# Attention in pairs of heads: the next pair's first and left-over scores ahead of the last pair's transposes

## The chip, the cores and the metric

One core of one Trainium2 chip runs the whole program. The metric is the device time of one execution in microseconds (us). Before the change it was 721.33 us, the median of three runs (720.55 to 721.36). For this kernel a difference of about 0.2%, 1.44 us, is what a measurement can tell from no change.

## What is computed

```python
def reference(q, k, v, U, V, w1, w2, w_in, w_sp, b_sp, w_out):     # B=4, H=8, S=576, D=64
    s = (q @ k.T) / sqrt(D) - slope[h] * abs(i - j)                # kept for 0 <= i - j < 128, else -1e9
    x = softmax(s) @ v                                             # heads side by side: (B, S, 512)
    u = x + (x.T @ U @ V).T                                        # mixing over the sequence, rank 32
    y = u + relu(u @ w1) @ w2                                      # 512 -> 2048 -> 512
    a, g = split(relu(y @ w_in))                                   # 512 -> 2 x 512
    return (a * (w_sp @ norm(g) + b_sp)) @ w_out
```

The change concerns the first line of it and the work woven into it: the attention with its window of 128 keys.

## The kernel before

The program is written engine by engine: five instruction streams, each in a fixed order of its own, with semaphores between them. Nothing reorders them. PE is the tensor engine, DVE the vector engine, ACT the scalar engine, POOL the gpsimd engine, SP the queue that issues the DMAs.

The attention goes in 16 steps, one for each pair of heads of each of the four batches, numbered p = 0 to 15 here (`step(b, i)` with p = 4b + i, from L1833 on PE and from L1312 on DVE; batches 2 and 3 are a hardware loop). A pair's 576 queries are cut into nine score tiles, `TILE_ORDER`: tiles 0 to 3 (blocks 0 and 1 of both heads) come from `scores_x`, tile 4 (the left-over 64 queries of both heads in one tile) from `scores_z`, tiles 5 to 8 from `scores_y`, which writes into the same two PSUM banks as `scores_x`. `scores_x` and `scores_y` use two halves of 64 rows of the PE array side by side; `scores_z`, the transposes and the mixing use all of its rows and columns; `values` uses two halves of 64 columns.

For each tile DVE adds the bias, takes the row's minimum of the negated scores and writes the tile to `sc` (`score`, L1258), and ACT takes the exponential (L927). PE then transposes the tiles in four groups of four (`turn` with f = 0 to 3, L1757). The groups use two PSUM banks in turn: f = 0 and 2 use bank 3, f = 1 and 3 use bank 4. DVE copies groups 0, 1 and 3 out (`keep_pt`, L1267), ACT copies group 2 (L936), and `turn` 2 and 3 wait for the copies of 0 and 1. `values` (L1774, L1781) multiplies the copies by v, `turn_back` (L1792) and `turn_x` (L1804) turn the result twice, with DVE dividing by the sums in between (`normalise`, L1288 and L1291). `mix_up` (L1827, L1828) and, once a batch, `mix_down` (L1813, L1814) do the low-rank mixing; `mix_up` uses the banks of the transposes and so waits for their copies. In the step after a `mix_down`, DVE has one more instruction, `lo_t` (L1298), ahead of `normalise`.

The work is staggered: a step p holds the scores of pair p, the transposes and `values` of pair p-1, and `turn_back`, `normalise` and `turn_x` of pair p-2. In the order of the code a step on PE before is: `turn` 0, `turn` 1 (p-1), `scores_x`, `scores_z` (p), `turn` 2 (p-1), `turn_back` (p-2), `turn` 3 (p-1), `scores_y` (p), `turn_x` (p-2), `mix_up`, `values` (p-1). On DVE it is: copies 0 and 1 (p-1), `score` tiles 0 to 3 (p), `lo_t` where there is one, `normalise` (p-2), copy 3 (p-1), `score` tiles 4 to 8 (p), the additions of the mixing, the sums.

The waits that matter are: `scores_x` waits until DVE has read all nine tiles of the pair before, since it writes over them; `scores_y` waits until DVE has read tiles 0 to 3 of its own pair, for the same reason; DVE's tile 0 waits for `scores_x`.

After the attention come the two large products (L1916 to L1918 and L1958 to L1960) and the second block (from L2027), in which PE is never without work for long.

Of the kernel before, what the change touches and what calls it, by code (L numbers as in the profile page):

```python
# [54 lines left out]
AFTER_X, AFTER_Z = 4, 5  # L55
# [70 lines left out]
def program(nc, qk, v_n, mu, mv, w1, w2, w_in, w_sp, b_sp, w_out, out_t, u_scr, r_scr, w2_scr, x2_scr, wc_scr):  # L126
    ctx = ExitStack()
    with ctx:
# [1110 lines left out]
        def _(dve):  # L1239
            def score(b, i, ns):  # L1240

                p, s = b * PAIRS + i, i % 2
                for n in ns:
                    t, e = TILE_ORDER[n]
                    if n in (0, AFTER_X, AFTER_Z):
                        dve.wait_ge(qk_done, 3 * p + (0, AFTER_X, AFTER_Z).index(n) + 1)
                    if n == 0 and not (isinstance(b, int) and p < 2):
                        dve.wait_ge(tr_done, 4 * (p - 1))
                    if n in (0, AFTER_X, AFTER_Z):
                        dve.sem_inc(dve_passed, 1)  # L1250
                    if e is None:
                        src, add, out = z_ps[:, 0:TAILKEYS], tbias[:, i, :], sc[:, s, n, 0:TAILKEYS]
                    elif t == 0:
                        src, add, out = s_ps[e][:, 0:P], bias[:, 2 * i + e, P:KEYS], sc[:, s, n, P:KEYS]
                    else:
                        c = {1: P, 2: 0, 3: KEYS}[t]
                        src, add, out = s_ps[e][:, c:c + KEYS], bias[:, 2 * i + e, :], sc[:, s, n, :]
                    dve.tensor_tensor_reduce(out=out, in0=src, in1=add, scale=-SCALE, scalar=3e38, op0=ALU.add,  # L1258
                                             op1=ALU.min, accum_out=mn[:, s, n:n + 1]).then_inc(scored, 1)

            def keep_pt(b, i, f):

                p = b * PAIRS + i
                dve.wait_ge(tr_done, 4 * p + f + 1)
                if f == 0 and not (isinstance(b, int) and p == 0):
                    dve.wait_ge(pv_done, p)
                dve.tensor_copy(pt[:, f % 2, f // 2 * BANK:(f // 2 + 1) * BANK],  # L1267
                                pt_ps[f % 2][:, :]).then_inc(pt_kept, 1)
# [43 lines left out]
            def step(b, i):  # L1312
                whole = not isinstance(b, int)
                one, two = whole or b * PAIRS + i >= 1, whole or b * PAIRS + i >= 2
                ago, k = MIX_STEP[i]
                if one:
                    keep_pt(*back(b, i, 1), 0)
                    keep_pt(*back(b, i, 1), 1)
                score(b, i, range(0, AFTER_X))
                if i == 2 and (whole or b >= 1):  # L1320
                    lo_t(b - 1)
                if two:
                    normalise(*back(b, i, 2))
                if one:
                    keep_pt(*back(b, i, 1), 3)
                score(b, i, range(AFTER_X, NT))
                if whole or b >= ago:
                    add_u(b - ago, k, pt_ps)
                if one:
                    sums(*back(b, i, 1))  # L1330
# [380 lines left out]
        def _(pe):  # L1711
            def scores_x(b, i):

                p, s = b * PAIRS + i, i % 2
                pe.wait_ge(qk_in[s], 32 * (b * 2 + i // 2 + 1))
                if not (isinstance(b, int) and p == 0):
                    pe.wait_ge(scored, p * NT)
                for t in (0, 1):
                    for e in range(2):
                        half = slice(e * D, (e + 1) * D)  # L1720
                        o = s_ps[e][:, 0:P] if t == 0 else s_ps[e][:, P:P + KEYS]
                        last = pe.matmul(o, qkraw[half, s, S + t * P:S + (t + 1) * P],  # L1722
                                         qkraw[half, s, 0:P if t == 0 else KEYS], start=True, stop=True)
                last.then_inc(qk_done, 1)

            def scores_z(b, i):

                s = i % 2
                pe.matmul(z_ps[:, 0:TAILKEYS], qkraw[:, s, S + (TILES - 1) * P:2 * S + TAIL],
                          qkraw[:, s, S - TAILKEYS:S], start=True, stop=True).then_inc(qk_done, 1)  # L1730
# [13 lines left out]
            def turn(b, i, f, mixed=None):  # L1744

                p = b * PAIRS + i
                pe.wait_ge(exp_done, p * NT + FILL_TILES[f])
                if f == 0 and not (isinstance(b, int) and p == 0):
                    pe.wait_ge(pt_third, p)
                elif f == 1 and not (isinstance(b, int) and p == 0):  # L1750
                    pe.wait_ge(pt_kept, 3 * p)
                elif f >= 2:
                    pe.wait_ge(pt_kept, 3 * p + f - 1)
                if f < 2 and mixed is not None:
                    pe.wait_ge(u_kept, mixed)
                for j, (n, w) in enumerate(FILLS[f]):
                    last = pe.transpose(pt_ps[f % 2][:, j * P:(j + 1) * P], sc[:, i % 2, n, w * P:(w + 1) * P],  # L1757
                                        ident[:, :])
                last.then_inc(tr_done, 1)
# [70 lines left out]
            def back(b, i, n):  # L1830
                return (b, i - n) if i >= n else (b - 1, i - n + PAIRS)

            def step(b, i):  # L1833
                whole = not isinstance(b, int)
                p = b * PAIRS + i
                one, two = whole or p >= 1, whole or p >= 2
                ago, k = MIX_STEP[i]
                last_ago, last_k = MIX_STEP[(i - 1) % PAIRS]
                last_ago += i == 0
                mixed = HEADROOM + (b - last_ago) * 2 * KD + 2 * last_k + 2 if whole or b >= last_ago else None  # L1840
                if one:
                    turn(*back(b, i, 1), 0, mixed)
                    turn(*back(b, i, 1), 1, mixed)
                scores_x(b, i)
                scores_z(b, i)
                if one:
                    turn(*back(b, i, 1), 2)
                if two:
                    turn_back(*back(b, i, 2))
                if one:  # L1850
                    turn(*back(b, i, 1), 3)
                scores_y(b, i)
                if two:
                    turn_x(*back(b, i, 2))
                if whole or b >= ago:
                    pe.wait_ge(pt_third, p)
                    pe.wait_ge(pt_kept, 3 * p)
                    mix_up(b - ago, k, pt_ps)
                if one:
                    values(*back(b, i, 1))  # L1860
                if i == 1 and (whole or b >= 1):
                    mix_down(b - 1)
# [280 lines left out]
```

## Time and profile before

| | us |
|---|---|
| median of three runs | 721.33 |
| the profiled execution, its time | 721.14 |
| its span, first to last instruction | 719.4 |
| PE busy | 708.4 |
| DVE busy | 452.4 |
| ACT busy | 339.0 |
| POOL busy | 179.6 |

The attention takes the first 137 us or so of the span. The timelines merge neighbouring instructions of one line into one row; the first number is the start, the second the time from the first one's start to the last one's end, and the ends of matmuls are modelled, so that the next row often starts before the last has ended. An fp32 matmul of the code stands as two in the trace. The distance between two starts is what a piece of work costs PE.

### The profile page before, as it was taken

To read this page: it belongs to the slowest core of one execution; us is meant where nothing else is said; L and a number is where in the kernel's file an instruction comes from. 1 tells how busy PE (TensorE), PEld (TensorE's weight loads), DVE (VectorE), ACT (ScalarE), POOL (GpSimd) and SP (SyncE) were. 2 spreads that over 40 slices of the span, in tenths; PEclk is the share of its full clock that TensorE was granted. 3 is DMA by queue.
4 is the path that set the end of the run, shared out by engine and by line. 5 is a ranking of instruction groups with operands and counts; after the bars stand their busy time and mean duration, and the time that the engine had idled before them with its cause. 6 is when DMAs were issued, how large, how long until landed. Compare 5 with 4: busy or idle time off the path is not lost.

```text
span 719.4 us, 13038 instructions
## 1 busy us (share of the span) xinstructions
PE 708.4 (98%) x4656; PEld 663.3 (92%) x4656; DVE 452.4 (63%) x1032; ACT 339.0 (47%) x764; POOL 179.6 (25%) x184
## 2 busy tenths in 40 slices
PE   8999999999999999999999999999999999999998
PEld 5677777799999999999999999999898998998997
DVE  6978787788673265248878976976384454354341
ACT  6878788865352243334444444444352432432422
POOL 2598646510009806660050000000010100100100
PEclk9999999999999999999999999999999999999999
DMA  7669974055457855899286175468900100100101
GB/s 224 192 212 389 355 262 144 16 177 189 176 171 260 300 205 181 285 370 374 87 277 220 44 264 176 149 208 301 335 1 1 67 0 0 66 0 0 66 1 67
DMA packets 72145, 122.46 MB, mean 170 GB/s; under 512 B 4896, under 2 KB 43808, under 8 KB 71584
## 3 DMA queue, kind: packets, MB, share of 16 engines
q1 hardware_dynamic: 72096, 121.82, 49.0%
q8 instruction: 29, 0.48, 0.3%
q14 instruction: 20, 0.16, 0.1%
HBM read 74.29 MB, written 47.51 MB: 169 GB/s over the span
## 4 chain that ended last, share of the span: by engine, by line
PE 74%; DVE 4%; ACT 0%; issue 0%; DVEq 0%
PE bank L1916 8%; PE bank L1918 8%; PE bank L1917 8%; PE bank L1958 4%; PE bank L1960 4%; PE bank L1959 4%; PE wide L1958 3%; PE wide L1960 3%; PE wide L1959 3%; PE bank L2067 2%; PE bank L2069 2%; PE bank L2068 2%; PE bank L1883 2%; PE bank L1881 2%; PE bank L1882 2%; PE wide L1882 2%
## 5 line engine op out<-in xcount | busy, mean ns | idle before, releaser
L1916 PE MATMUL bank<-xs,w1s 128*128 128x384 f32 x336 | 113.0, 336 | 1.0 <-DVE tok L1440 0.8
L1918 PE MATMUL bank<-xs,w1s 128*128 128x384 f32 x336 | 112.3, 334 | 0.0
L1917 PE MATMUL bank<-xs,w1s 128*128 128x384 f32 x336 | 112.3, 334 | 0.0
L1073 ACT ACTIVATE rk<-tok 128x768 fp32r<-128x768 f32 x72 | 61.0, 849 | 71.1 <-PE bank L1960 32.4
L914 POOL TENSOR_TENSOR vl<-vr,vh 128x512 fp32r<-128x512 f32 x8 | 11.2, 1405 | 291.8 <-ACT vh L1198 291.8
L1051 ACT ACTIVATE sums_u<-bank 128x384 f32<-128x384 f32 x72 | 35.3, 491 | 89.8 <-PE bank L1918 89.5
L927 ACT ACTIVATE sc<-sc,mn 128x256 f32<-128x256 f32 (+1 forms) x144 | 67.0, 468 | 19.7 <-DVE mn L1258 19.7
L1958 PE MATMUL bank<-rk,w2q 128*128 128x384 f32 x208 | 69.9, 336 | 0.2 <-DVE rk L1462 0.2
L1959 PE MATMUL bank<-rk,w2q 128*128 128x384 f32 x208 | 69.5, 334 | 0.0
L1960 PE MATMUL bank<-rk,w2q 128*128 128x384 f32 x208 | 69.5, 334 | 0.0
L1916 PEld LDWEIGHTS bank<-xs,w1s 128*128 128x128 f32 x336 | 63.1, 188 | 2.7 <-issue 1.3
L1917 PEld LDWEIGHTS bank<-xs,w1s 128*128 128x128 f32 x336 | 63.1, 188 | 0.0
L1918 PEld LDWEIGHTS bank<-xs,w1s 128*128 128x128 f32 x336 | 63.1, 188 | 0.0
L1462 DVE TENSOR_TENSOR rk<-tok,rk 128x768 fp32r<-128x768 f32 x48 | 46.8, 978 | 14.0 <-ACT rk L1073 13.6
L1258 DVE CUSTOM_DVE_ANT_0 sc<-bank,bias 128x256 f32<-128x256 f32 (+1 forms) x128 | 42.2, 384 | 5.8 <-PE bank L1722 4.9
L1958 PE MATMUL wide<-rk,w2q 128*128 128x384 f32 x128 | 42.9, 335 | 0.0
L1960 PE MATMUL wide<-rk,w2q 128*128 128x384 f32 x128 | 42.8, 334 | 0.0
L1959 PE MATMUL wide<-rk,w2q 128*128 128x384 f32 x128 | 42.8, 334 | 0.0
L1267 DVE COPY pt<-bank 128x512 f32<-128x512 f32 x48 | 31.4, 682 | 14.7 <-PE bank L1757 14.6
L1958 PEld LDWEIGHTS bank<-rk,w2q 128*128 128x128 f32 x208 | 39.0, 188 | 1.2 <-DVE rk L1462 1.1
L1959 PEld LDWEIGHTS bank<-rk,w2q 128*128 128x128 f32 x208 | 39.0, 188 | 0.0
L1960 PEld LDWEIGHTS bank<-rk,w2q 128*128 128x128 f32 x208 | 39.0, 188 | 0.0
(216 smaller groups left out, 1839.3 us busy)
## 6 DMA issues: line engine op xcount, KB each, us to landing
r_scr<-tok SPq DMA_DIRECT2D x20, 768.0 KB, 3.8
tok<-r_scr SPq DMA_DIRECT2D x15, 768.0 KB, 6.8
w1raw<-w SPq DMA_DIRECT2D x32, 256.0 KB, 4.1
w2q<-w_scr SPq DMA_DIRECT2D x4, 2048.0 KB, 10.3
wc_scr<-wprep SPq DMA_DIRECT2D x12, 512.0 KB, 6.5
w_scr<-tok SPq DMA_DIRECT2D x11, 512.0 KB, 3.1
qkraw<-qk SPq DMA_DIRECT2D x16, 320.0 KB, 4.9
qkraw<-qk SPq DMA_DIRECT2D x16, 288.0 KB, 3.5
```

The lines of the kernel that those rows point to most:

```text
L927: act.activation(w, w, ACT.Exp, bias=mn[:, s, n:n + 1], scale=-1.0, accum_out=sm[:, i, c:c + 1]).then_inc(exp_done, 1)
L1051: act.activation(sums_u[:, i, :], a_ps[s % 2][:, 0:HT], ACT.Copy).then_inc(kept, 1)
L1073: act.activation(rk[:, n % RING, 0], raw(g, RAW_OF[m])[:, 2 * j:2 * j + 2, :], ACT.Relu if m <= 3 else ACT.Copy).then_inc(rk_hi, 1)
L1258: dve.tensor_tensor_reduce(out=out, in0=src, in1=add, scale=-SCALE, scalar=3e38, op0=ALU.add, op1=ALU.min, accum_out=mn[:, s, n:n + 1]).th ...
L1267: dve.tensor_copy(pt[:, f % 2, f // 2 * BANK:(f // 2 + 1) * BANK], pt_ps[f % 2][:, :]).then_inc(pt_kept, 1)
L1462: dve.tensor_tensor(lo, x, hi, ALU.subtract).then_inc(rk_lo, 1)
L1916: pe.matmul(o, wh, ah, start=(k == 0 and m in FRESH), stop=False, skip_group_check=True)
L1917: pe.matmul(o, wl, ah, start=False, stop=False, skip_group_check=True)
L1918: last = pe.matmul(o, wh, al, start=False, stop=(k == 1), skip_group_check=True)
L1958: pe.matmul(o, wh, rh, start=(kk == 0 and m in FRESH), stop=False, skip_group_check=True)
L1959: pe.matmul(o, wl, rh, start=False, stop=False, skip_group_check=True)
L1960: last = pe.matmul(o, wh, rl, start=False, stop=(kk == UNITS - 1), skip_group_check=True)
```

## The change

On PE, `scores_x` and `scores_z` of the step now stand ahead of the transposes of the pair before, and `turn` 2 stands behind `turn_back`. On DVE, `score` of tiles 0 and 1 stands ahead of the first two copies, and tiles 2 and 3 stay behind them. ACT, POOL and SP have the same instructions in the same order, and none is added or removed but a few register instructions of the loop.

```diff
@@ DVE, step
                 ago, k = MIX_STEP[i]
+                score(b, i, range(0, 2))
                 if one:
                     keep_pt(*back(b, i, 1), 0)
                     keep_pt(*back(b, i, 1), 1)
-                score(b, i, range(0, AFTER_X))
+                score(b, i, range(2, AFTER_X))
@@ PE, step
+                scores_x(b, i)
+                scores_z(b, i)
                 if one:
                     turn(*back(b, i, 1), 0, mixed)
                     turn(*back(b, i, 1), 1, mixed)
-                scores_x(b, i)
-                scores_z(b, i)
-                if one:
-                    turn(*back(b, i, 1), 2)
                 if two:
                     turn_back(*back(b, i, 2))
                 if one:
+                    turn(*back(b, i, 1), 2)
                     turn(*back(b, i, 1), 3)
                 scores_y(b, i)
```

PE in step 7, from `values` of one step to `turn_x` of the next, before (L1757 are the transposes of the scores, L1722 is `scores_x`, L1729 `scores_z`, L1739 `scores_y`):

```order
L1757 MATMUL bank<-ident,sc 128x128 x8
L1722 MATMUL bank<-qkraw 128x128 x2
L1722 MATMUL bank<-qkraw 128x256 x2
L1729 MATMUL bank<-qkraw 128x192
L1757 MATMUL bank<-ident,sc 128x128 x4
L1792 MATMUL wide<-ident,xt 128x128 x4
L1792 MATMUL wide<-ident,xt 64x128
L1757 MATMUL bank<-ident,sc 128x128 x4
L1739 MATMUL bank<-qkraw 128x256 x4
L1804 MATMUL wide<-ident,xn 128x128 x5
```

The same in the changed kernel, where each of these lines has a number one higher:

```order
L1723 MATMUL bank<-qkraw 128x128 x2
L1723 MATMUL bank<-qkraw 128x256 x2
L1730 MATMUL bank<-qkraw 128x192
L1758 MATMUL bank<-ident,sc 128x128 x8
L1793 MATMUL wide<-ident,xt 128x128 x4
L1793 MATMUL wide<-ident,xt 64x128
L1758 MATMUL bank<-ident,sc 128x128 x8
L1740 MATMUL bank<-qkraw 128x256 x4
L1805 MATMUL wide<-ident,xn 128x128 x5
```

The three rows of scores moved to the front, and the second and third group of transposes now stand together behind `turn_back`.

DVE in step 6, the one after the first `mix_down`, before (COPY is `keep_pt`, L1258 with a bank is `score`, L1298 `lo_t`, L1288 the start of `normalise`):

```order
L1267 COPY pt<-bank 128x512 x2
L1258 ISA sc,mn<-bank,bias 128x128
L1258 ISA mn 128x1
L1258 ISA sc,mn<-bank,bias 128x128
L1258 ISA mn 128x1
L1258 ISA sc,mn<-bank,bias 128x256
L1258 ISA mn 128x1
L1258 ISA sc,mn<-bank,bias 128x256
L1258 ISA mn 128x1
L1298 TENSOR_TENSOR tst<-wide,tst 64x512
L1288 TENSOR_TENSOR xn<-wide,rinv 128x512
```

The same in the changed kernel:

```order
L1258 ISA sc,mn<-bank,bias 128x128
L1258 ISA mn 128x1
L1258 ISA sc,mn<-bank,bias 128x128
L1258 ISA mn 128x1
L1267 COPY pt<-bank 128x512 x2
L1258 ISA sc,mn<-bank,bias 128x256
L1258 ISA mn 128x1
L1258 ISA sc,mn<-bank,bias 128x256
L1258 ISA mn 128x1
L1298 TENSOR_TENSOR tst<-wide,tst 64x512
L1288 TENSOR_TENSOR xn<-wide,rinv 128x512
```

The first two scores stand ahead of the two copies; the other two stay directly ahead of `lo_t` and `normalise`.

PE in step 1, the second pair, where there is no pair p-2 yet; first before, from `scores_y` of step 0 on:

```order
L1739 MATMUL bank<-qkraw 128x256 x4
L1757 MATMUL bank<-ident,sc 128x128 x8
L1722 MATMUL bank<-qkraw 128x128 x2
L1722 MATMUL bank<-qkraw 128x256 x2
L1729 MATMUL bank<-qkraw 128x192
L1757 MATMUL bank<-ident,sc 128x128 x8
L1739 MATMUL bank<-qkraw 128x256 x4
```

And in the changed kernel:

```order
L1740 MATMUL bank<-qkraw 128x256 x4
L1723 MATMUL bank<-qkraw 128x128 x2
L1723 MATMUL bank<-qkraw 128x256 x2
L1730 MATMUL bank<-qkraw 128x192
L1758 MATMUL bank<-ident,sc 128x128 x16
L1740 MATMUL bank<-qkraw 128x256 x4
```

The first eight transposes, which stood ahead of the second pair's scores, now stand behind them, and all sixteen follow each other.

## Rows read from the trace of the kernel before

**Rows 1.** The page, its head: span and instructions.

```profile
span 719.4 us, 13038 instructions
```

**Rows 2.** Busy time by stretch: us, PE, PEld, DVE, ACT, POOL, clock, DMA share, GB/s.

```profile
9.00:33.00 24.00, 21.63 (x196) 16.02 (x194) 22.87 (x93) 20.60 (x74) 8.75 (x10) 1.00 0.66 203
33.00:137.00 104.00, 103.60 (x902) 80.65 (x897) 83.38 (x336) 85.29 (x278) 68.86 (x59) 1.00 0.71 244
...
144.00:719.00 575.00, 570.32 (x3493) 557.33 (x3492) 338.35 (x574) 224.55 (x399) 93.21 (x97) 1.00 0.45 157
```

**Rows 3.** Timeline of PE, plain step: start us, us, engine, line, operation, operands.

```profile
101.71 1.09 PE L1757 MATMUL bank<-ident,sc 128*128 128x128 f32 x8
102.74 0.93 PE L1722 MATMUL bank<-qkraw 64*128 64x128 f32 x8
103.59 0.59 PE L1729 MATMUL bank<-qkraw 128*128 128x192 f32 x2
104.02 0.60 PE L1757 MATMUL bank<-ident,sc 128*128 128x128 f32 x4
104.46 0.71 PE L1792 MATMUL wide<-ident,xt 128*128 128x128 f32 x5
105.00 0.60 PE L1757 MATMUL bank<-ident,sc 128*128 128x128 f32 x4
105.53 1.14 PE L1739 MATMUL bank<-qkraw 64*128 64x256 f32 x8
...
107.12 0.38 PE L1827 MATMUL bank<-mvh,tst 128*128 128x288 f32 x1
...
109.71 0.55 PE L1757 MATMUL bank<-ident,sc 128*128 128x128 f32 x3
```

**Rows 4.** Timeline of DVE, same step; in brackets idle time and what ended it.

```profile
102.41 1.29 DVE L1267 COPY pt<-bank 128x512 f32<-128x512 f32 x2 [0.48 <-PE bank L1757]
103.97 0.29 DVE L1258 CUSTOM_DVE_ANT_0 sc<-bank,bias 128x128 f32<-128x128 f32 x1 [0.27 <-PE bank L1722]
...
104.74 0.42 DVE L1258 CUSTOM_DVE_ANT_0 sc<-bank,bias 128x256 f32<-128x256 f32 x1
105.09 0.08 DVE L1258 DVE_READ_ACCUMULATOR2_ANT mn<- 128x1 f32 x1
105.44 0.69 DVE L1288 TENSOR_TENSOR xn<-wide,rinv 128x512 f32<-128x512 f32 x1 [0.27 <-PE wide L1792]
...
106.24 0.67 DVE L1267 COPY pt<-bank 128x512 f32<-128x512 f32 x1
```

**Rows 5.** Timeline of DVE in the step after `mix_down`.

```profile
88.84 0.69 DVE L1298 TENSOR_TENSOR tst<-wide,tst 64x512 fp32r<-64x512 f32 x1
89.57 0.69 DVE L1288 TENSOR_TENSOR xn<-wide,rinv 128x512 f32<-128x512 f32 x1
```

**Rows 6.** Timeline of PE in that step.

```profile
85.48 1.03 PE L1757 MATMUL bank<-ident,sc 128*128 128x128 f32 x8
...
90.50 0.76 PE L1804 MATMUL wide<-ident,xn 128*128 128x128 f32 x5
```

**Rows 7.** Timeline of PE, second pair's step.

```profile
11.06 0.93 PE L1722 MATMUL bank<-qkraw 64*128 64x128 f32 x8 [0.35 <-DVE mn L1258]
...
13.43 1.13 PE L1739 MATMUL bank<-qkraw 64*128 64x256 f32 x8
```

**Rows 8.** Timeline of DVE, second to fourth step.

```profile
14.77 0.42 DVE L1258 CUSTOM_DVE_ANT_0 sc<-bank,bias 128x256 f32<-128x256 f32 x1 [0.38 <-PE bank L1739]
...
17.58 1.29 DVE L1267 COPY pt<-bank 128x512 f32<-128x512 f32 x2
...
26.95 1.29 DVE L1267 COPY pt<-bank 128x512 f32<-128x512 f32 x2
...
29.39 0.08 DVE L1258 DVE_READ_ACCUMULATOR2_ANT mn<- 128x1 f32 x1
```

**Rows 9.** Timeline of PE, fourth step: scores that had waited for DVE.

```profile
29.52 1.13 PE L1739 MATMUL bank<-qkraw 64*128 64x256 f32 x8
```

## The prediction

> **What bounds the kernel now.** I read the span [rows 1], then the busy time by stretch [rows 2]. From 33 to 137 us PE is busy 103.60 of 104 us and DVE 83.38: the attention's steady part is bound by PE. From 9 to 33 us DVE is busy 22.87 of 24 us and PE 21.63: there DVE sets the pace. Behind 144 us PE is busy 570.32 of 575 us with work that the change doesn't touch. So the attention's length goes into the total nearly one for one, and the question is what a step costs after the change.
>
> Next the timelines of one plain step. A step before takes 109.71 - 101.71 = 8.00 us, and no PE row of it names a wait [rows 3]. DVE in the same step has two holes, 0.48 us ahead of the first copies and 0.27 us ahead of the first score [rows 4]. DVE's last score of tiles 0 to 3 ends at 105.09 + 0.08 = 105.17, and PE needs it for `scores_y`, which starts at 105.53: a cover of only 0.36 us. That cover is where the change bites.
>
> **The change part by part, plain step.** I count from U, the start of `scores_x`, which now opens the step.
>
> PE's own time up to `scores_y`, by distances between starts [rows 3]: `scores_x` 0.85, `scores_z` 0.43, four transposes 0.44, four more 0.44, `turn_back` 0.54, four transposes 0.44, and the last four with the passage to the half-array scores 0.53. Sum 3.67. Before, `scores_y` stood 105.53 - 101.71 = 3.82 behind the step's start. The 0.15 saved is one passage between forms of matmul: `values` (64 columns), transposes (whole array), `scores_x` (64 rows) were two passages; `values` to `scores_x` is one. The trace has no passage from 64 columns to 64 rows. From below its cost beyond normal spacing is zero, from above the two that it replaces, about 0.25 (a passage costs about 0.1 where I can read it: 0.53 for the last four transposes against 0.44). I take the same 0.1, because both known kinds cost that.
>
> Row and rule: the rows show a later start at every passage between forms. The Trainium skill, "TensorEngine Tiling (Array Packing)", section Key Properties, says that changing the tiling mode drains the TensorE, whichever tile is used; by that rule alone, one passage fewer in a step, the change would be a gain, and the rows agree with the rule. What it leaves out is the wait that follows.
>
> DVE's chain in the same step. Tiles 0 and 1 can start when `scores_x` is through: U + 0.93, and DVE starts 0.30 later (102.74 + 0.93 = 103.67 against 103.97) [rows 3, 4], so U + 1.23. The two take 0.43 (104.74 less 103.97, less one of 0.35 for tile 2) and end at U + 1.66. The first copy needs transpose group 0: 0.85 + 0.43 + 0.60 = U + 1.88, plus 0.05 from transposes to copy (half of the eight of 101.71 ends at 102.36, the copy starts at 102.41), so U + 1.93. DVE idles 0.27 here. Two copies occupy 2 x 0.61 (the pair of 1.29 less one of 0.67 is the distance) [rows 4]: tile 2 starts at U + 3.14, tile 3 at 3.48, its end with the accumulator's read is at 3.83 + 0.08 = U + 3.91. PE answers DVE's end after 0.05 (29.39 + 0.08 against 29.52) [rows 8, 9]. So `scores_y` starts at **U + 3.96**: 0.29 later than PE could, and 0.14 later than before. The cover of 0.36 has become a wait, since copies 0 and 1, which ran while PE did `scores_x`, now stand between `scores_x` and tiles 2 and 3.
>
> Behind `scores_y` everything on PE keeps its distances, if nothing else is late. `mix_up` would start 107.12 - 105.53 = 1.59 later, at U + 5.55. It needs the third copy: `normalise` starts near U + 3.9, the copy 0.80 later, and it lasts 0.67 [rows 4], so U + 5.37: in time by 0.18. The earlier start of ACT's exponentials of tiles 0 and 1 buys nothing: ACT's copy of group 2 waits for transposes that come at U + 3.1, and tile 4's exponential stands behind work that waits for `turn_x`. A plain step costs **+0.14**. There are seven with `mix_up` (7 to 9, 11 to 13, 15): +0.98. Steps 4 and 5 without it have the same chain up to `scores_y`; one of them loses a small wait, so +0.23 for both.
>
> **The step after a `mix_down`** (6, 10 and 14). Before, it starts at 85.48, and `turn_x` at 90.50, 5.02 later, comes 0.93 after the start of `normalise` (89.57), which comes 0.73 after `lo_t` (88.84) [rows 5, 6]. It already hangs on DVE. No passage is saved here, because `mix_down` uses the whole array: `scores_x` starts 0.09 behind the point where the transposes stood. Then tile 3 ends as above at 3.83 (accumulator's start), `lo_t` 0.12 later, `normalise` + 0.73, `turn_x` + 0.93: 0.09 + 3.83 + 0.12 + 0.73 + 0.93 = 5.70, against 5.02: +0.68. The 0.12 may vanish or not (it stands between the read and `lo_t` and is idle), so 0.56 to 0.68. I take 0.65, three times: **+1.95**.
>
> **The start.** Step 1's `scores_x` waits for DVE's ninth score and starts at 11.06 either way [rows 7]. Before, the first eight transposes and DVE's copies of them were done beside that wait. After, transposes start at 11.06 + 1.28 = 12.34, the first copy at 12.34 + 0.65 = 12.99, tile 2 at 14.20, tile 3 ends at 14.97, `scores_y` starts at 15.02, against 13.43 [rows 7]: +1.59. DVE's next scores follow 1.34 behind `scores_y` (14.77 against 13.43) [rows 7, 8], so all of it passes on. In step 2, DVE is free at 17.58 + 1.59 = 19.17 [rows 8] and again waits 0.27 between its first scores and first copy, which costs some 0.2 more; in step 3 it is free long after PE (26.95, [rows 8]), the order of its work doesn't matter, and 0.1 comes back. Sum for steps 1 to 3: **+1.68**.
>
> Total: 1.68 + 0.23 + 1.95 + 0.98 = **+4.84 us**. Behind step 15 the tail has its old order, and the 575 us that follow are PE's. The profiled execution took 721.14 us for a span of 719.4, 0.19 below the median of 721.33. So 721.14 + 4.84 = 725.98; I give 726.0.
>
> **Rivals.**
>
> Not slower: the passage decides. If DVE's chain kept up, PE would gain 0.15 to 0.2 in the twelve steps whose predecessor ends with `values`, 1.8 to 2.4 us, against the start's 1.7: 721.14 - 0.7 to 721.14 - 0.1, about 720.7. For this, tile 3 must end at U + 3.62 and not at 3.91. Against it: the 1.88 to the end of group 0 and the 1.22 of the copies are plain rows. I give 0.09, a third of it faster by over 0.2%.
>
> Milder: the plain steps break even (the new passage costs nothing), and `lo_t` follows at once: 1.5 + 3 x 0.5 = 3.0, less what a step may gain; 722.8 to 724.2. Chance 0.10.
>
> Dearer: the register instructions that the loop puts between tile 1 and the first copy, or the third copy with its cover of 0.18, hold up every step by a further 0.3: twelve steps, +3.6, 729.6. Chance 0.06.
>
> The clock: a step would have 21 transposes in a row, 2.4 us; the granted clock is 1.00 in every stretch of the attention, 2.4 GHz, with eight in a row [rows 2]. If it fell to 1.2 GHz in each such run, a run would at most double: 15 x 2.4 = +36, 757. Nothing in the rows speaks for it, and PE does the same work in between; chance 0.01. The Trainium skill, "TensorE: Matmul & The Clock Gate", Part 4, says that matmuls in transpose mode don't count as a busy PE for the clock; no row here shows such a fall.
>
> That the change does something else than it says is out: the order of the instructions shows it.
>
> **How the numbers follow.** The forecast has 0.74, with its own range of 724.3 to 728.4: from below, +3.3 (a free passage at the nine plain steps and 0.2 less at the start and at `lo_t`); from above, +7.2 (a passage of 0.2, and 0.1 of register work, in twelve steps). The range that should hold the time 8 times in 10 takes part of the milder rival: 723.4 to 728.6. A measurement of this kernel tells 0.2%, 1.44 us, from no change. Slower by more: 0.91 (forecast, dearer, clock, milder). Within: 0.06. Faster by more: 0.03.
>
> **What the profile after would show.** In a plain step of 8.14 us, a wait of PE for DVE's `mn` ahead of `scores_y`, which starts 3.96 behind `scores_x`; DVE idle 0.3 us between tile 1 and the first copy, and about 1 us ahead of tile 0; `turn_x` in steps 6, 10 and 14 some 5.6 behind `scores_x`, with a wait for `xn`; `scores_y` of step 1 at 15.0. The attention's end, the first large product, some 4.8 us later than before, and the same distances from there on. I am wrong if `scores_y` stands at U + 3.7, if the start is made up in steps 2 and 3, or if PE's waits behind the attention shrink.

## The result, and the profile after

The changed kernel takes **728.07 us** (median of four runs, 726.98 to 729.25) against 721.35 (720.55 to 722.18) of the kernel before, measured beside it: a ratio of 1.0096, with a 95% interval of 1.0082 to 1.011. It is slower by 0.8 to 1.1%, and the forecast of 726.0 in 723.4 to 728.6 holds the time, near its upper end. The profiled execution took 726.98 us.

The page's head and the busy time by stretch, columns as in [rows 2]:

```profile
span 725.2 us, 13044 instructions
```

```profile
9.00:33.00 24.00, 21.10 (x168) 15.80 (x169) 20.47 (x80) 18.90 (x65) 8.77 (x10) 0.93 0.59 186
33.00:137.00 104.00, 101.83 (x871) 77.36 (x870) 80.11 (x327) 82.99 (x267) 67.35 (x58) 1.00 0.72 247
```

The span is 5.8 us longer than in [rows 1], and PE's instructions are the same but for their order. In the stretch from 33 to 137 us PE is busy 101.83 us where it was 103.60 [rows 2]: it now waits where it didn't. The first stretch has a clock of 0.93, where before it was 1.00.

The plain step of PE that answers to [rows 3]:

```profile
97.86 0.93 PE L1723 MATMUL bank<-qkraw 64*128 64x128 f32 x8
...
101.81 1.13 PE L1740 MATMUL bank<-qkraw 64*128 64x256 f32 x8
...
106.00 0.93 PE L1723 MATMUL bank<-qkraw 64*128 64x128 f32 x8
```

`scores_y` stands 101.81 - 97.86 = 3.95 behind `scores_x`, and the step takes 106.00 - 97.86 = 8.14 us, where it took 8.00. DVE in the same step, answering to [rows 4]:

```profile
99.09 0.29 DVE L1258 CUSTOM_DVE_ANT_0 sc<-bank,bias 128x128 f32<-128x128 f32 x1 [0.99 <-PE bank L1723]
...
99.78 1.29 DVE L1267 COPY pt<-bank 128x512 f32<-128x512 f32 x2 [0.19 <-PE bank L1758]
...
101.67 0.08 DVE L1258 DVE_READ_ACCUMULATOR2_ANT mn<- 128x1 f32 x1
```

DVE is idle 0.99 us ahead of tile 0 and 0.19 ahead of the copies; tile 3's read ends at 101.67 + 0.08 = 101.75, and `scores_y` starts 0.06 later. The idle time of PE ahead of the line of `scores_y`, over the whole attention: 5.5 us in 15 waits (from the view of that line):

```profile
  DVE mn L1258: 5.5, 15
```

That is 1.0 us in the first pair's step, which is in the kernel before too, and some 0.3 us in each of fourteen others.

The step after a `mix_down` (step 10), DVE and then PE, answering to [rows 5, 6]:

```profile
92.99 0.69 DVE L1298 TENSOR_TENSOR tst<-wide,tst 64x512 fp32r<-64x512 f32 x1
93.72 0.69 DVE L1288 TENSOR_TENSOR xn<-wide,rinv 128x512 f32<-128x512 f32 x1
```

```profile
89.06 0.93 PE L1723 MATMUL bank<-qkraw 64*128 64x128 f32 x8
...
94.65 0.77 PE L1805 MATMUL wide<-ident,xn 128*128 128x128 f32 x5 [0.50 <-DVE xn L1291]
```

`turn_x` starts 94.65 - 89.06 = 5.59 behind `scores_x`, 0.93 behind the start of `normalise` (93.72), which is 0.73 behind `lo_t`.

The start, PE in step 1, answering to [rows 7], and the busy time there in stretches of 2 us:

```profile
10.34 0.93 PE L1723 MATMUL bank<-qkraw 64*128 64x128 f32 x8 [1.81 <-DVE mn L1258]
...
11.62 3.71 PE L1758 MATMUL bank<-ident,sc 128*128 128x128 f32 x16
15.26 1.14 PE L1740 MATMUL bank<-qkraw 64*128 64x256 f32 x8
...
18.22 0.93 PE L1723 MATMUL bank<-qkraw 64*128 64x128 f32 x8
```

```profile
9.00:11.00 2.00, 0.66 (x8) 0.55 (x8) 1.19 (x8) 1.81 (x7) 0.00 (x0) 1.00 0.89 264
11.00:13.00 2.00, 2.00 (x13) 1.79 (x10) 0.83 (x5) 1.15 (x6) 0.00 (x0) 0.66 0.96 343
13.00:15.00 2.00, 1.98 (x10) 1.47 (x9) 1.74 (x6) 0.36 (x1) 0.00 (x0) 0.50 0.09 33
```

This isn't in the forecast. The granted clock falls to 0.50, the lower of the two levels, from 11.66 to 15.07 us in the record of the clock, and the sixteen transposes take 3.71 us. Before it, PE had been idle for 1.81 us, up to 10.34, in a stretch in which it had little work anyway.

The waits of PE, longest sums first (line waited at, what for, us in total, times, longest):

```profile
PE wide L1805 <- DVE xn L1291: 2.1, 4, 0.6
...
PE wide L1793 <- ACT xt L945: 1.0, 3, 0.5
```

The three waits for ACT's `xt` lie in steps 2, 3 and 4; that of step 4 is the longest, 0.47 us.

### The profile page after: what moved, and what is told of

Same layout as the page of the kernel before. It is cut to its first block, busy times and chain, and to the rows that moved or that the text cites. A ratio compares the mean times of both kernels' runs of the same rounds, so it can differ in the third digit from the quotient of the medians.

```text
span 725.2 us, 13044 instructions
## 1 busy us (share of the span) xinstructions
PE 711.0 (98%) x4656; PEld 663.5 (91%) x4656; DVE 450.7 (62%) x1032; ACT 340.6 (47%) x764; POOL 179.6 (25%) x184
## 4 chain that ended last, share of the span: by engine, by line
PE 73%; DVE 5%; ACT 0%; issue 0%; DVEq 0%; ACTq 0%
PE bank L1916 8%; PE bank L1918 7%; PE bank L1917 7%; PE bank L1958 4%; PE bank L1960 4%; PE bank L1959 4%; PE wide L1958 3%; PE wide L1960 3%; PE wide L1959 3%; PE bank L2067 2%; PE bank L2069 2%; PE bank L2068 2%; PE bank L1883 2%; PE bank L1881 2%; PE bank L1882 2%; PE wide L1882 2%
## 5 line engine op out<-in xcount | busy, mean ns | idle before, releaser
L1258 DVE CUSTOM_DVE_ANT_0 sc<-bank,bias 128x256 f32<-128x256 f32 (+1 forms) x128 | 43.3, 383 | 24.2 <-PE bank L1723 21.8
L1758 PE MATMUL bank<-ident,sc 128*128 128x128 f32 x256 | 37.2, 285 | 1.4 <-ACT sc L927 1.0
```

## Where the time went

A step's length is the distance between the starts of two steps: of `scores_x` after the change, and before it of `turn` 0 (in step 1 of `scores_x` there too). In the steps behind a `mix_down` the table counts, as the prediction did, the 0.09 us by which `scores_x` now starts later behind `mix_down`; "difference" is what all steps of a row lose together, in us:

| part | before | after | difference | forecast |
|---|---|---|---|---|
| up to `scores_x` of step 1 | 11.06 | 10.34 | -0.72 | 0 |
| step 1, `scores_x` to the next step | 5.33 | 7.88 | +2.55 | +1.59 |
| step 2 | 7.48 | 7.76 | +0.28 | +0.2 |
| step 3 | 9.31 | 9.26 | -0.05 | -0.1 |
| step 4 | 7.65 | 8.02 | +0.37 | } +0.23 |
| step 5 | | | +0.13 | } |
| steps 6, 10, 14 | | | +0.54, +0.65, +0.63 | 3 x 0.65 |
| steps 7 to 9, 11 to 13, 15 (a plain one takes) | 8.00 | 8.13 | +0.95 | +0.98 |
| up to the first large product | 143.96 | 149.31 | +5.35 | +4.84 |
| behind it | 575.44 | 575.89 | +0.45 | 0 |

The first row is no effect of the change. The first pair's `scores_x`, which has the same place in both kernels, took 1.65 us in the trace of before and 0.93 in that of after:

```profile
4.91 1.65 PE L1722 MATMUL bank<-qkraw 64*128 64x128 f32 x8
```

```profile
4.90 0.93 PE L1723 MATMUL bank<-qkraw 64*128 64x128 f32 x8
```

1.65 us is also what these matmuls take in a stretch with a clock of 0.50, and the record of the clock explains it. Its first entry, of 1.00, begins at 6.70 us in the trace of before and at 4.83 in that of after. Ahead of that entry nothing is recorded, and the views print 1.00 there all the same. In the fourteen traces of this case the entry begins between 4.74 and 7.32 us, and these matmuls take the longer the later it begins: 0.93 us up to 4.89, then 1.04 (5.18), 1.19 (5.50), 1.28 (5.69), 1.52 (6.16), and 1.65 from 6.47 on. So the row is the moment at which the full clock was granted, which differs from one execution to the next.

## The experiments

All kernels are the changed kernel with one or two edits, unless said otherwise; ratios are against the kernel before on the same chip.

**Step 1 in the old order.** Does the start cost what the sum says, and is the half clock part of it?

```diff
@@ PE, step
+                early = not whole and p == 1
+                if early:
+                    turn(*back(b, i, 1), 0, mixed)
+                    turn(*back(b, i, 1), 1, mixed)
                 scores_x(b, i)
                 scores_z(b, i)
-                if one:
+                if one and not early:
@@ DVE, step
-                score(b, i, range(0, 2))
+                early = not whole and b * PAIRS + i == 1
+                if not early:
+                    score(b, i, range(0, 2))
...
-                score(b, i, range(2, AFTER_X))
+                score(b, i, range(0 if early else 2, AFTER_X))
```

> The changed kernel with step 1 alone (the second pair) in the order of before, on PE and on DVE. Theory: the start costs 1.6 us by itself (scores and copies that no longer run beside the wait for DVE's ninth score) and some 1 us by a stretch of TensorE clock 0.50 that follows PE's idle time there. Both go: the clock is 1.00 throughout, the step's scores_y starts about 2.4 us behind its scores_x, and the time is before + 3.5 us (7 plain steps x 0.14, 3 steps after mix_down x 0.62, steps 4 and 5 together 0.5), about 724.9. Rival: the loss sits in the steady steps alone and the slow clock is chance: no better than before + 6.

Measured: 724.84 us (723.96 to 725.91, five runs), ratio 1.0055 (1.0041 to 1.0069). PE in step 1:

```profile
10.29 0.93 PE L1725 MATMUL bank<-qkraw 64*128 64x128 f32 x8 [0.36 <-DVE mn L1258]
...
12.66 1.13 PE L1742 MATMUL bank<-qkraw 64*128 64x256 f32 x8
...
15.62 0.93 PE L1725 MATMUL bank<-qkraw 64*128 64x128 f32 x8
```

`scores_y` is 2.37 behind `scores_x` and the next step begins 5.33 behind it, as before; the clock is 1.00 in all five runs. All later steps have the lengths of the changed kernel. Against the kernel before on its own chip this one loses 724.84 - 721.13 = 3.7 us, the changed kernel 6.7. So some 3.0 us of the loss lie in step 1 and 3.7 in the rest, where the forecast had 1.59 and 3.25.

**Only PE's order changed**, DVE's old one (both copies, then all four scores):

```diff
@@ DVE, step
-                score(b, i, range(0, 2))
                 if one:
                     keep_pt(*back(b, i, 1), 0)
                     keep_pt(*back(b, i, 1), 1)
-                score(b, i, range(2, AFTER_X))
+                score(b, i, range(0, AFTER_X))
```

> The new order on PE, the old order on DVE (two copies, then tiles 0 to 3). Theory: DVE's chain decides; tile 0 starts at U + 3.14 (U: start of scores_x), tile 3 ends at U + 4.34, scores_y starts at U + 4.39, a plain step takes 8.56 us, and the time is some 6 us above the changed kernel's, 733 to 735. Rival: what costs is PE's new order by itself (another passage between forms of matmul, more waits of turn_back): a plain step stays at 8.13 and the time at 728.

Measured: 733.97 us (a single run). A plain step of PE:

```profile
65.88 0.93 PE L1722 MATMUL bank<-qkraw 64*128 64x128 f32 x8
...
70.25 1.13 PE L1739 MATMUL bank<-qkraw 64*128 64x256 f32 x8 [0.39 <-DVE mn L1258]
...
74.43 0.93 PE L1722 MATMUL bank<-qkraw 64*128 64x128 f32 x8
```

`scores_y` stands at U + 4.37, the step takes 8.55, where adding the same rows in another order had given 4.39 and 8.56. That is the best evidence that the chain (transposes, copies, scores, `scores_y`) is the right one. A stretch at the lower clock is in this run's time too (its mean clock is 0.994), so the rows are compared and not the time.

**All four scores ahead of the copies** on DVE:

```diff
@@ DVE, step
-                score(b, i, range(0, 2))
+                score(b, i, range(0, AFTER_X))
                 if one:
                     keep_pt(*back(b, i, 1), 0)
                     keep_pt(*back(b, i, 1), 1)
-                score(b, i, range(2, AFTER_X))
```

> The changed kernel with DVE's tiles 0 to 3 all ahead of the two copies. If only the two scores behind the copies were at fault, scores_y would start at U + 3.67 and a plain step would take 7.85, and the time would be near 724. Theory: the copies are the length of the chain, wherever the scores stand; copy 1 ends at U + 3.63, transposes 3 follow it, scores_y starts at U + 4.25 and a plain step takes 8.4 to 8.5, 732 to 734.

Measured: 731.53 us (a single run, mean clock 0.995), a little below the range that was expected. The third group of transposes now waits for the first copy, as expected, and `scores_y` is at U + 4.27:

```profile
65.08 0.93 PE L1722 MATMUL bank<-qkraw 64*128 64x128 f32 x8
...
68.20 1.23 PE L1757 MATMUL bank<-ident,sc 128*128 128x128 f32 x8 [0.25 <-DVE pt L1267]
69.35 1.13 PE L1739 MATMUL bank<-qkraw 64*128 64x256 f32 x8
```

The plain step takes 8.45. Two scores ahead of the copies, as in the change, is the best of the three splits: 3.95 against 4.37 and 4.27.

**The clock.** The half clock followed an idle PE, so extra matmuls with results that nobody uses were put into the wait ahead of `scores_x` of step 1. Eight of them first:

```diff
@@ PE, ahead of step 1
                 if i == 1:
                     pe.wait_ge(dist_done, 3)
+                    for n in range(8):
+                        pe.matmul(t_ps[:, 0:KEYS], wst[:, 0, 0:P], wst[:, 0, :], start=True, stop=True)
```

> The changed kernel with eight more 256-column matmuls on zeros on PE ahead of step 1, into a bank that nothing reads then; the output is not touched. They fill most of PE's idle time ahead of the second pair's scores. Theory: PE's idle time there is what the fall of the clock to 0.50 follows, so the clock stays at 1.00, the sixteen transposes take 2.7 us and not 3.7, and the time is about 1 to 1.7 us below the changed kernel's, before + 5.0 to 5.7, with less spread between runs. Rival: the fall comes from the sixteen transposes in a row, or by chance: clock 0.50 in 11 to 15 us again, before + 6.5.

Measured: 728.38 us (728.21 to 729.1), ratio 1.0105 (1.0089 to 1.012). The clock stayed at 1.00 through step 1, but eight were too many: `scores_x` started only at 12.23 us, later by more than the half clock had cost. So the run says something on the clock and nothing on its price. The same with four:

> The changed kernel with four more 256-column matmuls on zeros on PE ahead of step 1 (eight held the second pair's scores up by 1.9 us: they started at 12.23 and not at 10.34). Four take 1.7 us and should end as DVE's ninth score does. Theory (the fall of the clock follows PE's idle time there): clock 1.00, second pair's scores at 10.3 to 10.4 (11.1 where the clock rises late), scores_y 3.95 behind them, time before + 5.0 to 5.7. Rival (the fall comes by chance or from the transposes in a row): a stretch at 0.50 again and before + 6.5 or more.

Measured: 726.67 us (726.49 to 727.78, four runs), ratio 1.0081 (1.0066 to 1.0096), clock 1.00 in each. PE in step 1 (L1871 are the extra matmuls):

```profile
9.19 1.99 PE L1871 MATMUL wide<-wst 128*128 128x256 f32 x8
11.11 0.93 PE L1723 MATMUL bank<-qkraw 64*128 64x128 f32 x8
...
15.06 1.14 PE L1740 MATMUL bank<-qkraw 64*128 64x256 f32 x8
```

`scores_x` starts at 11.11, close to its 11.06 in [rows 7] (in both traces the full clock came late), and `scores_y` 3.95 behind it, which is the chain of the prediction (3.96) without the slow clock. Step 1 takes 6.91 us here and 7.88 in the trace of the changed kernel: 0.97 us for the half clock. By the medians it is some 1.2 us, since this kernel loses 5.6 us against the one before and the changed kernel 6.7; with four runs of each the two intervals overlap, so the traces are the better measure.

**Copy 1 on ACT.** If DVE's two copies are what holds tiles 2 and 3 up, one copy less there must bring the plain step below the old one.

```diff
@@ DVE, step
                     keep_pt(*back(b, i, 1), 0)
-                    keep_pt(*back(b, i, 1), 1)
@@ ACT, step
                 exp_tiles(b, i, range(0, 2))
                 if not first or i >= 1:
+                    keep_pt(*back(b, i, 1), 1)
                     keep_pt(*back(b, i, 1), 2)
```

The last pair's copy behind step 15 moves to ACT too, and the counts that PE waits for are changed to fit; neither is shown.

> The changed kernel with copy 1 of the four copies of transposes moved from DVE to ACT, which is idle about 1 us there (with the semaphores counted anew). Theory: the chain scores, copy 0, copy 1, tiles 2 and 3 is what scores_y waits for; it gets 0.61 shorter, scores_y starts at U + 3.67, a plain step takes 7.85 us (0.15 below the kernel before: the one passage between forms of matmul fewer), turn_x in steps 6, 10 and 14 comes at U + 5.0; time 723 to 723.5, the start's loss is left. Rival: something else holds scores_y (the passage from 64 columns to 64 rows, the transposes' own pace): the plain step stays above 8.0 and the time above 726.

Measured: 725.99 us (723.68 to 727.25, five runs), ratio 1.0057 (1.0038 to 1.0075). PE and DVE in a plain step:

```profile
97.94 0.93 PE L1723 MATMUL bank<-qkraw 64*128 64x128 f32 x8
...
101.64 1.13 PE L1740 MATMUL bank<-qkraw 64*128 64x256 f32 x8
```

```profile
99.87 0.69 DVE L1269 COPY pt<-bank 128x512 f32<-128x512 f32 x1 [0.19 <-PE bank L1760]
...
101.16 0.08 DVE L1260 DVE_READ_ACCUMULATOR2_ANT mn<- 128x1 f32 x1
```

Tile 3 is read by 101.16 + 0.08 = 101.24, and PE doesn't need it before 101.64. `scores_y` is at U + 3.70, the step takes 7.88 (97.94 to 105.82). That is PE's own sum, 3.67 and one passage less than before: with its cover back, the new order *is* 0.12 us a step faster than the old. (The last experiment shows that the old order gains nothing from the same copy.) But the time was some 2.5 us above what was expected. In this kernel the lower clock came earlier and stayed longer:

```profile
9.00:11.00 2.00, 0.26 (x4) 0.00 (x0) 1.67 (x9) 1.58 (x8) 0.00 (x0) 0.72 0.75 137
11.00:13.00 2.00, 1.93 (x9) 1.31 (x10) 0.10 (x1) 1.00 (x5) 0.00 (x0) 0.50 1.02 389
...
15.00:17.00 2.00, 1.98 (x10) 1.45 (x8) 0.92 (x5) 1.09 (x2) 0.00 (x0) 0.57 0.00 0
```

Step 1 took 8.9 us. The five runs fall in two groups: two with a mean clock of 0.997 took 723.7 and 723.9 us, three with 0.995 took 726.0 to 727.3. Whether that is the reason was tested by putting the four extra matmuls into this kernel:

> The changed kernel with two edits: copy 1 on ACT in every step, and four extra matmuls with results that nobody uses put on PE between scores_y of step 0 and scores_x of step 1 (they fill the 1.81 us in which PE waits for DVE). Theory (the half clock follows PE's idle stretch; without it ACT's copy alone brings 723.0 to 723.5): clock 1.00 throughout in every run; scores_x of step 1 to that of step 2 some 6.5 us instead of the 8.9 of the run with ACT's copy alone, all later steps as there; 2.4 us less than that kernel's 725.99, so 723.2 to 723.9, and a spread of the single runs as narrow as that of the kernel before. Rival (the scatter of ACT's copy from 723.7 to 727.3 has another cause, in ACT or the DMAs): the clock is full but times still lie between 723.7 and 727, with a median of 725 or more.

Measured: 723.9 us (722.87 to 724.23, six runs), ratio 1.0034 (1.0022 to 1.0047), clock 1.00 in each. PE at the start of steps 1 and 2:

```profile
10.38 0.93 PE L1723 MATMUL bank<-qkraw 64*128 64x128 f32 x8
...
17.10 0.93 PE L1723 MATMUL bank<-qkraw 64*128 64x128 f32 x8
```

Step 1 takes 6.72 us. So the 2.1 us between the two kernels (2.2 in step 1) are the clock's. ACT's copy is worth some 3 us to the new order: 726.67 - 723.9 = 2.8 by the medians with the extra matmuls in both kernels, 5.6 - 2.5 = 3.1 against the kernel before on each one's chip.

**`lo_t` behind copy 3**, to bring `turn_x` of steps 6, 10 and 14 forward:

```diff
@@ DVE, step
-                if i == 2 and (whole or b >= 1):
-                    lo_t(b - 1)
                 if two:
                     normalise(*back(b, i, 2))
                 if one:
                     keep_pt(*back(b, i, 1), 3)
+                if i == 2 and (whole or b >= 1):
+                    lo_t(b - 1)
```

> The changed kernel with lo_t behind normalise and copy 3 on DVE. It is a look at steps 6, 10 and 14 alone. Theory: turn_x there waits for normalise, which waits for lo_t; it comes at U + 5.02 and not at U + 5.59. mix_up then waits for lo_t and starts at U + 6.0 instead of U + 6.19, so the time gains 0.6 us at most, 727.4. Rival: turn_x waits for something else: it stays at U + 5.59.

Measured: 729.69 us (a single run). The expectation failed. DVE and PE in step 10:

```profile
95.22 0.27 DVE L1291 TENSOR_TENSOR xn<-wide,rinv 64x128 f32<-64x128 f32 x1
95.42 0.67 DVE L1267 COPY pt<-bank 128x512 f32<-128x512 f32 x1
96.12 0.69 DVE L1298 TENSOR_TENSOR tst<-wide,tst 64x512 fp32r<-64x512 f32 x1
```

```profile
96.96 0.74 PE L1805 MATMUL wide<-ident,xn 128*128 128x128 f32 x5 [1.07 <-DVE tst L1298]
```

`normalise` is done at 95.5, and yet `turn_x` starts at 96.96, behind `lo_t`. In these steps `turn_x` writes into the bank out of which `lo_t` reads, so it waits for both, whatever their order; late, `lo_t` has copy 3 in front of it too. I had read `turn_x`'s wait in [rows 5, 6] as one for `normalise` alone. Each of the three steps is 0.42 to 0.45 us longer than in the changed kernel. Ahead of step 6 PE also waited 1.65 us for the loads of q and k. SP had issued the two transfers at 47.0 and 47.5 us, and the later one took 7.1 us to land (who waited for them, and the time from issue to landing):

```profile
  PE bank L1723: 1.6, 1
...
DMA to landing us min/median/max: 4.2/5.7/7.1
```

The step before it is 1.8 us longer by that. No run ties this wait to the order on DVE; the landing times differ between kernels (see the last section).

**The three edits together** (step 1 in the old order, copy 1 on ACT, `lo_t` late):

> Step 1 in the old order, copy 1 on ACT, lo_t behind copy 3, the rest as in the changed kernel. Theory: 7 plain steps x -0.15 against the kernel before, steps 6, 10 and 14 -0.15 to -0.2 each, steps 2 and 3 +0.3 for turn_back's wait for ACT, steps 4 and 5 about 0: before - 1.0 to - 1.5 us, 719.6 to 720.1. Rival: ACT with one copy more becomes the bound (it was busy 6.8 us of each 8 and waits for turn_x): plain steps above 8.0 and no gain over the kernel before.

Measured: 724.87 us (724.19 to 726.14, five runs), ratio 1.0053 (1.0039 to 1.0067), some 5 us above what was expected. The plain steps are 7.88, but `lo_t` costs as above, and in step 1 the fourth group of transposes waits for ACT's copy, which stands behind ACT's exponentials:

```profile
13.66 0.63 PE L1762 MATMUL bank<-ident,sc 128*128 128x128 f32 x4 [1.07 <-ACT pt L936]
```

**Step 1 in the old order and copy 1 on ACT, without that wait.** In step 1 ACT does the copy ahead of its exponentials (the edit is shown against the kernel with copy 1 on ACT; step 1 on PE and DVE is as in the first experiment):

```diff
@@ ACT, step
+                early = first and i == 1
+                if early:
+                    keep_pt(*back(b, i, 1), 1)
                 exp_tiles(b, i, range(0, 2))
                 if not first or i >= 1:
-                    keep_pt(*back(b, i, 1), 1)
+                    if not early:
+                        keep_pt(*back(b, i, 1), 1)
                     keep_pt(*back(b, i, 1), 2)
```

> The changed kernel with two edits: step 1 (the second pair) keeps the order of the kernel before on PE and DVE, and the copy of transpose group 1 is ACT's in every step; in step 1 ACT does it ahead of its exponentials of tiles 0 and 1, in all other steps behind them. Theory (what the change costs is DVE's copies 0 and 1 between PE's first scores and tiles 2 and 3, and at the start the lost cover): plain steps 7.88, so 7 x -0.12 = -0.84 against before; steps 6, 10 and 14 at 8.22, level with before; steps 2 to 4 as in the run with ACT's copy alone (8.08, 8.88, 8.35 against 7.48, 9.31, 7.65), +0.9; step 1 at 5.3 to 5.5 and no wait of 1.07 for ACT's copy. Sum about 0: 720.6 to 721.9, the same as before. Rival (something else in the new order costs time, so that ACT's copy doesn't cure it): 724 and more.

Measured: 722.37 us (721.59 to 724.76, twelve runs), ratio 1.0018 (1.0008 to 1.0027). All of the loss but 0.2% is gone (the expectation's upper end was 721.9), so the start and the copy in DVE's chain are nearly all that the change had cost. Against the trace of before, this one is 0.9 us late at the start of step 5, wins back 0.2 in the ten steps up to step 15, and loses 0.4 in the tail, where PE now waits 0.16 us for ACT's `xt`. Two of PE's waits (steps 2 to 4 above all):

```profile
PE wide L1801 <- ACT xt L945: 1.2, 4, 0.5
...
PE bank L1766 <- ACT sc L927: 1.0, 2, 0.6
```

ACT, now with a copy more, is what is late there.

The same with steps 1 to 3 in the old order, ACT's copy 1 ahead of its exponentials in all three:

> As the kernel with step 1 in the old order and ACT's copy of group 1, but steps 1, 2 and 3 all have first transposes ahead of first scores on PE and copies ahead of the scores on DVE, with ACT's copy of group 1 ahead of its exponentials there. Theory (in steps 1 to 3 DVE sets the pace, and the new order only adds its hole between the first scores and the first copy): steps 2 and 3 at 7.5 and 8.7 and not 8.08 and 8.88; 0.5 to 0.8 us faster than that kernel, 720.0 to 721.3. Rival (ACT, busy 20.6 of 24 us there, becomes late when its copy stands first, and transposes 3 wait for it): no gain over that kernel, 721.3 to 722.5.

Measured: 721.86 us (721.19 to 722.46, eleven runs), ratio 1.0006 (0.9998 to 1.0015). Half a microsecond better than the last one, the least that was expected, though the two intervals overlap; the time itself missed its range of 720.0 to 721.3 and lies in that of the rival. It is level with the kernel before, not ahead of it. What the start gained (step 5 starts 0.9 us earlier than in the last kernel) was mostly given back at step 6, where PE waits for q and k. SP had issued the later transfer 0.7 us earlier than in the kernel before, but it took 6.4 us to land instead of 5.8:

```profile
51.60 0.93 PE L1729 MATMUL bank<-qkraw 64*128 64x128 f32 x8 [0.70 <-DMA qkraw<-qk]
```

**The kernel before, with copy 1 on ACT.** Is ACT's copy a gain by itself? ACT does it ahead of its exponentials in every step.

> The kernel before, old order everywhere, with one edit: copy 1 is ACT's, ahead of its exponentials of tiles 0 and 1. Theory (in the old order PE's plain step is bound by PE alone, so that a copy less on DVE is worth nothing there; it is worth something where PE waits for DVE, in the steps after a mix_down and at the start): plain steps 8.00 still, steps 6, 10 and 14 shorter by 0.4 to 0.6 each, steps 1 to 3 shorter by 0.5 to 1 in all: 718.8 to 719.8. If the copy is a gain in every step whatever the order, plain steps would be 7.88 too, 718.0. Rival (ACT is late: its copy waits for transposes 1 while exponentials stand behind it): 721.4 to 724, with waits of PE for ACT's sc or pt.

Measured: 721.85 us (721.13 to 722.57, eleven runs), ratio 1.001 (1.0001 to 1.0019): no gain. DVE at the start of step 10, before and with the copy moved:

```profile
86.12 1.29 DVE L1267 COPY pt<-bank 128x512 f32<-128x512 f32 x2 [2.86 <-PE bank L1757]
87.61 0.29 DVE L1258 CUSTOM_DVE_ANT_0 sc<-bank,bias 128x128 f32<-128x128 f32 x1 [0.20 <-PE bank L1722]
```

```profile
85.98 0.69 DVE L1273 COPY pt<-bank 128x512 f32<-128x512 f32 x1 [2.72 <-PE bank L1763]
87.48 0.29 DVE L1264 CUSTOM_DVE_ANT_0 sc<-bank,bias 128x128 f32<-128x128 f32 x1 [0.80 <-PE bank L1726]
```

In the old order the copies end before `scores_x` is through, so a copy less only lengthens the idle time ahead of tile 0, from 0.20 to 0.80 us. The chain that ends in `turn_x` begins at `scores_x`, and `turn_x` stands 90.37 - 85.35 = 5.02 behind the step's start, as in [rows 6]. I had expected 0.4 to 0.6 us there and another 0.5 to 1 at the start, 718.8 to 719.8 in all, and that was wrong: an engine that sets a time need not do so with all its instructions.

## The prediction, point by point

- **Plain steps, right.** Forecast `scores_y` at U + 3.96 and a step of 8.14; measured 3.95 and 8.13 to 8.14. The assumed cost of the passage from 64 columns to 64 rows (as much as the known ones) is borne out where nothing covers it: with ACT's copy the step is PE's alone and 0.12 shorter than before, where the prediction's 0.15 came from one passage less. The rule of the Trainium skill, "TensorEngine Tiling (Array Packing)", section Key Properties, that a change of tiling mode drains the engine, agrees with that; by itself it would have forecast a gain.
- **Steps after a `mix_down`, right in size.** Forecast `turn_x` 5.61 behind `scores_x` (the sum of 5.70 counts from 0.09 earlier) and +0.65; measured 5.59 and +0.54 to +0.65. The chain named there (`lo_t`, `normalise`, `turn_x`) was right in its order only: with `lo_t` late it turned out that `turn_x` waits for `lo_t` itself too.
- **Step 1: mis-sized.** The forecast of +1.59 holds at the full clock (`scores_y` 3.95 behind `scores_x` with the four extra matmuls). The 0.96 us on top is the half clock. The step of the prediction that failed is "`scores_x` waits and starts at 11.06 either way": true, but before, PE had transposes to do during this wait, and now it has nothing for 1.81 us. An idle stretch was counted as free because it costs nobody any time; it cost the clock. That `scores_y` of step 1 came at 15.26, close to the forecast 15.0, is luck: the step began 0.72 us early by the first row of the table and lasted 0.96 longer than forecast.
- **The clock rival, right kind, wrong place.** It was looked for in 21 transposes in a row, in all steps. There the clock is 1.00 throughout. By the Trainium skill, "TensorE: Matmul & The Clock Gate", Part 4, transposes don't count as a busy PE in the same way as other matmuls; the plain steps, with 21 of them in a row between other matmuls, show no fall (1.00 from 33 to 137 us). The fall came in the one step in which PE was idle beforehand. Whether the sixteen transposes behind the wait took part in it was not separated.
- **Steps 4 and 5: one wait missed.** +0.50 instead of +0.23. `turn_back` now stands ahead of transposes 2, 0.60 us earlier in the step (2.15 us behind its start in step 5, where it was 2.75), and in steps 2 to 4 it meets ACT's copy `xt` before that is done: 1.0 us in three waits. The prediction followed DVE and let ACT's copies be; they had no row ahead of it.
- **Behind the attention, +0.45**, forecast as nothing. Most of it is one wait of 0.34 us for DVE's `xs` at 277 us, in the first large product. Five of the fourteen traces have this wait, and in them this part, whose code is the same in all, lasts 575.8 to 576.0 us; in the nine without it, that of before among them, it lasts 575.4 to 575.6. Why the wait comes in some and not in others stays open.
- **Between median and profile.** The forecast was made against the profiled execution. There it missed by 1.0 us (726.98 against 725.98): half clock +0.96, steps 4 and 5 +0.27, behind the attention +0.45, less the 0.72 of the table's first row. That the early start took back most of the half clock is luck, and the miss of the median, 2.1 us, took most of the range's margin. The median is 1.1 us above that execution; the changed kernel's mean clocks were 0.998, 0.997, 0.998 and 0.995, and the run with 0.995 is the slowest (729.25), so part of this may be a longer time at the lower clock.
- The rival "not slower" fell by the 3.95; "milder" fell too, though ACT's copy shows what it would have looked like; "dearer" (register work, third copy) shows nowhere in the traces.
- Slips in the prediction's sums, none of which moves the forecast: steps 1 to 3 add up to 1.69, not 1.68; eleven steps, not twelve, follow a step that ends with `values`; the clock rival's +36 was added to the old time.

## What to carry to other kernels

Before work that runs beside a wait is moved behind it, write down when the next engine will need its result: here DVE's copies had run beside PE's first scores, and 1.2 us of them went into a chain with 0.36 us to spare. Then look at what PE does during the wait instead; if it is nothing, the clock may fall (here in 11 of 12 runs, at a cost of 1.0 to 2.2 us in the traces). And a shorter list of work on an engine helps only where that work lies on the chain from its latest input.

## What the hardware showed

- **The clock fell in a stretch of little work, without a long idle time.** PE was idle for 0.7 to 1.0 us ahead of the first pair's `scores_y` and for 1.81 us ahead of step 1. 11 of 12 runs (of the changed kernel and of four variants of it) had a mean clock under 0.999, and their traces show one stretch at 0.50, 3.41 us long in the changed kernel and 6.83 in three variants. It began 1.3 us behind the end of the wait in the changed kernel (11.66 us), and inside the wait in the variants (9.88 with ACT's copy, 10.60 and 10.65 in the two with single runs). Of 58 runs of the eight variants with work in that place, none had a mean clock under 0.999. The fall is likely then, not certain: the variant with `lo_t` late kept a clock of 1.00 through the same 1.81 us. At the lower clock transposes stood about twice as far apart (ten from 13 to 15 us, 0.20 us each, against 0.11 in [rows 3]), and the stretch cost 1.0 us in the changed kernel and 2.2 in the one with ACT's copy.
- **The start of the full clock moves between executions.** It was recorded from 4.74 to 7.32 us in the fourteen traces, and up to 0.72 us of the time of one execution hang on it.
- **Price of a passage between forms of matmul**: one fewer in a step gave 0.12 us.
- **A load's time from issue to landing isn't fixed.** The later of the two transfers of q and k for step 6 landed 4.4 us behind its issue in the changed kernel, 5.8 in the kernel before, 6.4 with steps 1 to 3 in the old order and 7.1 with `lo_t` late. PE waited 0.3 to 1.65 us for it in five variants; two of these had only come there earlier than the kernel before, so what a faster start gains is in part given back at this load. What makes the landing late was not tested.
